# A delta-rule attention kernel with two feed-forward layers: the prologue of its first group on seven PSUM banks, x of the second layer in a buffer of its own, and group 1's key products kept in one piece

## What is computed

```python
def _attn_ref(q, k, v, beta):            # 4 x 8 heads, 768 steps, head size 48
    k_n = k / (np.linalg.norm(k, axis=-1, keepdims=True) + 1e-06)
    state = np.zeros((B, H, D, D))
    for t in range(S):
        kt, vt, bt = (k_n[:, :, t], v[:, :, t], beta[:, :, t, None])
        y[:, :, t] = np.einsum('bhd,bhde->bhe', q[:, :, t], state)
        v_old = np.einsum('bhde,bhd->bhe', state, kt)
        state = state + bt[:, :, :, None] * np.einsum('bhd,bhe->bhde', kt, vt - v_old)
    return y

x = heads side by side                   # 3072 tokens x 384
h = np.maximum(x @ w_in, 0.0)            # 384 -> 2048
x = h * h @ w_out                        # 2048 -> 384
gate = 1.0 / (1.0 + np.exp(-(x @ w_gate)))   # 384 -> 1536
y = gate * (x @ w_val) @ w_out2          # 1536 -> 384
```

## Time and profile before

| | us |
|---|---|
| median of 3 runs | 1003.74 |
| the runs | 1003.34 to 1004.78 |
| profiled execution, device time | 1005.03 |
| its span (first to last instruction) | 1003.3 |
| PE busy | 951.6 |
| DVE busy | 657.3 |
| ACT busy | 513.2 |

### The profile page before, as it was taken

How to read it: one execution, slowest core, us unless ns; L and a number is a source line. 1 busy time by engine, 2 the same in 40 slices (tenths; PEclk the granted TensorE clock), 3 DMA queues, 4 the chain that set the end, 5 groups by cost and what they waited for, 6 DMA issues and landing times.

```text
span 1003.3 us, 24593 instructions
## 1 busy us (share of the span) xinstructions
PE 951.6 (95%) x10354; PEld 523.5 (52%) x10354; DVE 657.3 (66%) x1261; ACT 513.2 (51%) x898; POOL 13.2 (1%) x27
## 2 busy tenths in 40 slices
PE   2876999999999999999999989999999999999998
PEld 1464465465456556546544435555555555555554
DVE  6978957957875794795334674575666665756745
ACT  4874666666476575646649943323233333232332
POOL 0000000000000000000000000000000000000000
PEclk7867999999999999999999999999999999999999
DMA  9516015115104201400215010010010010010000
GB/s 311 123 35 127 2 34 111 49 31 123 42 3 97 64 34 35 95 33 3 96 36 211 7 63 1 2 63 0 0 63 0 0 63 0 22 41 0 32 1 32
DMA packets 21001, 52.23 MB, mean 52 GB/s; under 512 B 2672, under 2 KB 12912, under 8 KB 20528
## 3 DMA queue, kind: packets, MB, share of 16 engines
q1 hardware_dynamic: 20320, 50.60, 18.1%
q10 hardware_dynamic: 592, 0.33, 0.2%
HBM read 41.48 MB, written 9.44 MB: 51 GB/s over the span
## 4 chain that ended last, share of the span: by engine, by line
PE 87%; DVE 6%; issue 3%; ACT 2%; DMA 1%; SPq 0%; POOL 0%; DVEq 0%; POOLq 0%
PE psum L673 74%; PE psum L587 3%; PE psum L518 1%; PE psum L544 1%; DMA raw_a<-in_w_in 1%; PE psum L531 1%; PE psum L574 1%; PE psum L602 1%; PE psum L556 1%; ACT w L900 1%; PE psum L616 1%; DVE attn L1192 1%; PE psum L483 1%; ACT w L806 1%; DVE work L1234 1%
## 5 line engine op out<-in xcount | busy, mean ns | idle before, releaser
L673 PE MATMUL psum<-work,w 128*128 128x512 f16 x1728 | 389.3, 382 | 12.2 <-issue 6.2
L673 PE MATMUL psum<-work,attn 128*128 128x512 f16 (+1 forms) x1836 | 367.6, 360 | 0.0
L673 PEld LDWEIGHTS psum<-work,attn 128*128 128x128 f16 x1836 | 179.5, 98 | 182.6 <-DVE work L1234 1.3
L673 PEld LDWEIGHTS psum<-work,w 128*128 128x128 f16 x1728 | 164.9, 98 | 209.3 <-issue 13.6
L806 ACT ACTIVATE work<-work 128x512 f16<-128x512 f32 (+1 forms) x264 | 155.7, 624 | 154.5 <-DVE work L1402 151.5
L1402 DVE SCALAR_TENSOR_TENSOR work<-psum,work 128x512 f32<-128x512 f32 x72 | 49.7, 691 | 134.5 <-PE psum L673 120.3
L1214 DVE SCALAR_TENSOR_TENSOR work<-work 128x512 f16<-128x512 f16 x96 | 66.2, 690 | 61.3 <-ACT work L806 59.6
L806 ACT ACTIVATE work<-psum,scal 128x512 f32<-128x512 f32 x90 | 60.1, 682 | 81.7 <-PE psum L673 81.6
L806 ACT ACTIVATE attn<-psum 64x384 f32<-64x384 f32 (+5 forms) x160 | 65.9, 441 | 66.3 <-PE psum L544 34.9
L806 ACT ACTIVATE work<-psum 128x512 f32<-128x512 f32 x96 | 57.1, 595 | 64.6 <-PE psum L673 63.3
L806 ACT ACTIVATE w<-w 128x1024 f16<-128x1024 f32 x36 | 38.0, 1057 | 72.6 <-DVE w L1418 72.6
(11 more groups left out here) (112 smaller groups left out, 713.7 us busy)
## 6 DMA issues: line engine op xcount, KB each, us to landing
attn<-in_kt SPq DMA_DIRECT2D x24, 192.0 KB, 4.4
attn<-in_v SPq DMA_DIRECT2D x24, 192.0 KB, 4.7
attn<-in_kn SPq DMA_DIRECT2D x24, 192.0 KB, 3.9
x_spill<-work SPq DMA_DIRECT2D x6, 768.0 KB, 3.4
xt<-x_spill SPq DMA_DIRECT2D x6, 768.0 KB, 5.0
attn<-in_qt SPq DMA_DIRECT2D x20, 192.0 KB, 4.3
y_out<-work SPq DMA_DIRECT2D x5, 768.0 KB, 3.6
work<-in_w_out SPq DMA_DIRECT2D x1, 3072.0 KB, 24.2
```

Of the source, the lines that this page charges most:

```text
L673: m = mm(dst, x, z, start=first and i == 0, stop=last and i == len(a) - 1)
```

## The change

- **Banks.** In stage 0 all fills but group 1's kk choose among seven banks (5, 6, 7, 2, 3, 4, 1), always the one that was filled longest ago; later stages and group 1's kk keep three. Banks 1 to 4 also serve the pieces of w_in's low part, so the first attention fill in each shared bank waits until all 12 pieces are copied out (`PIECE_SHARED`).
- **Group 1's key products.** Chunk by chunk, one product of 64 rows per pair instead of two of 32 (`HALVED` is empty). They stand between the pieces: 8 pieces, chunk 0, 2 pieces, chunk 1, 2 pieces. Read out in one piece each before (128x512), they now take four instructions per bank, as group 0's do.
- **Order of stage 0.** qk of chunk 0 ahead of mid; mid, off and `place_e` chunk by chunk; qk of chunk 1 is filled at step 9 and read at step 11. `cut_out`, `cut_small` and `first_weights_out` move. Twenty-five fillers stand behind five named fills instead of eight single ones ahead of fills.
- **x of group 0.** Its maximum is taken per chunk. ACT writes the three high parts, DVE only the low ones.
- **Loads.** SP issues group 1's keys ahead of v, q and k of group 0.
- **Stages 1 to 5.** Places move by a few steps, and so do the elimination columns.
- **Stage 6.** The second layer's weights are prepared in blocks 0 to 13 instead of 0 to 15, and its first x is split at block 12 into a buffer of its own (`x2_hi`, `x2_lo`, in the attention's memory), without the wait for the last `hidden`. The second layer reads x from there throughout.

```diff
+NB_FIRST = 7
-PLACE = dict(rows=6, scale_v=8, mid=(8, 11), off=(10, 14), qk=(-4, 10), ks=(8, 15), dr=(11, 16), grow=(13, 20), xt=(18, 21), xmax=23, xscale=27, xsplit=31, kk=(3, 5), lanes=14, norm=15, start=15)
+PLACE = dict(rows=7, scale_v=7, mid=(8, 11), off=(10, 15), qk=(-3, 10), ks=(7, 15), dr=(11, 17), grow=(13, 23), xt=(19, 25), xmax=26, xscale=27, xsplit=31, kk=(4, 5), lanes=7, norm=13, start=13)
+    _n = NB_FIRST if _s == 0 and (_kind, _g) != ("kk", 1) else NB
+    _b = min(range(_n), key=lambda b: _last[b])
...
-HALVED = (1,)
+HALVED = ()
-REST_FIRST = 12
+REST_AT = {OPEN: (0, 1, 2, 3, 4, 5, 6, 7), 0: (8, 9), 1: (10, 11)}
-WARM_AHEAD = ("mid", "off", "qk", "ks", "dr")
+WARM_BEHIND = {("mid", 0, 0): 4, ("mid", 1, 1): 1, ("dr", 1, 1): 4, ("su", 1, 1): 2, ("xt", 1, 1): 14}
...
-        a_bank = [psum[:, b, :] for b in (5, 6, 7)]
+        a_bank = [psum[:, b, :] for b in (5, 6, 7, 2, 3, 4, 1)]
...
+        x2_hi, x2_lo = (xs2[:, i * KC * TOK:(i + 1) * KC * TOK].rearrange("p (k t) -> p k t", k=KC) for i in (0, 1))
...
             def open_fill(*f):
+                if f in PIECE_SHARED:
+                    pe.wait_ge(w_lo_done, REST_PIECES)
...
+            def first_high_parts():
+                act.wait_ge(x_scaled, 5)
+                act.wait_ge(w_small_done, 1)
+                act.wait_ge(w_out_done, 1)
+                for kc in range(KC):
+                    run(x_hi[:, kc], xt32[:, TOK * kc:TOK * (kc + 1)], scale=cell(X + 2)).then_inc(x_cut, 1)
...
             def second_weights(k):
-                if k == 14:
+                if k == 10:
                     scale_x2(0)
...
+                if k == 12:
+                    split_x(x2_split, GROUPS, x2_hi, x2_lo)
...
-                    if s == GROUPS and step == place(s, "xsplit") + 1:
-                        dve.wait_ge(h_full, N1 * GROUPS)
-                        split_x(x2_split, GROUPS)
```

More of the change, by code:

```diff
@@ L137, in column_steps @@
     start, end = place(g - 1, "start") + 1, place(g, "rows")
-    steps = [(g - 1, step) for step in range(start, STEPS)]
+    steps = [(g - 1, step) for step in range(start, STEPS if g > 1 else place(0, "xsplit"))]
     steps += [(g, step) for step in range(0, end)]
@@ L654, in attention @@
                         turn(g, c, x)
+                    if s == 0:
+                        keep_clock(WARM_BEHIND.get((kind, c if kind not in ("mid", "off") else x, x), 0) if g == 0 else 0)
             def rest_of_first(n):
@@ L710, in stage @@
                     attention(s, step)
-                    if s == 0 and step == OPEN:
-                        for n in range(REST_FIRST):
-                            rest_of_first(n)
-                    for n in range(REST_FIRST, REST_PIECES):
-                        if s == 0 and step == place(0, "rest")[n - REST_FIRST]:
+                    if s == 0:
+                        for n in REST_AT.get(step, ()):
                             rest_of_first(n)
@@ L990, in stage @@
                         weight_root(1, WO)
-                        for n in range(REST_FIRST):
-                            cut_rest_first(n)
-                    if s == 0 and step == 0:
-                        place_e(0)
-                    for n in range(REST_FIRST, REST_PIECES):
-                        if s == 0 and step == place(0, "rest")[n - REST_FIRST]:
+                    if s == 0:
+                        for n in REST_AT.get(step, ()):
                             cut_rest_first(n)
@@ L1002, in stage @@
                             cut_small(n)
-                    if s < GROUPS - 1 and step == place(s, "norm"):
+                    if s < GROUPS - 1 and step == place(s, "norm" if s else "root"):
                         root_k(s + 1)
@@ L1342, in stage @@
                         scale_v(s)
-                    for f in FILL_AT.get((s, step), []):
+                    for f in READ_AT.get((s, step), []):
                         evacuate(*f)
+                    if s == 0 and step == place(0, "first_max"):
+                        max_of_chunk(0)
                     if chain and step == place(s, "xmax"):
```

161 lines of the change are left out of this document (102 added, 59 removed).

## The result

The changed kernel takes **995.1 us** (median of 6 runs, 994.0 to 999.2); the kernel before, run beside it, took 1003.86 (6 runs, 1002.6 to 1004.8). The ratio is 0.9919, with an interval of 0.9907 to 0.9932: 7 to 9 us faster. The profiled execution took 994.02, with a span of 992.2 instead of 1003.3. It was the fastest of its kernel, and that of before (1005.03) was slower than all six runs of its own, so the 11.1 us between the two traces are about 2.3 more than the medians show.

The account below looks back on a forecast made before the run. PE was taken to bound the kernel from the first `hidden` on, so the end moves with that start and seam losses: -4.6 - 0.4 + 0.3 + 0.2 = -4.5, from 1003.74 to 999.2; range 993.0 to 1003.3.

Parts of the forecast that it names:

- First qk at 49.2: Prologue: qk waits for all 12 pieces paced by ACT, starting 4.5 earlier; longer key read-out costs 2.8 on the path.
- qk to su of chunk 0: Prologue: PE's clock decides; 21.9 to 71.1 at the lower level, 13.6 with pauses to 62.8 at the upper.
- From su to the first `hidden`: Prologue: 7.0 to 7.7 to dr of chunk 1, 7.4 to 8.1 to the last xt, then 6.0.
- The clock: Prologue: PE near clock 0.5 for 13 to 17 us from 49 or 53 on.
- 90.0 for the first `hidden`: End of the prologue: taken between 88.6 and 92.0 for low spells of 13 and 17 us; 4.6 earlier.
- Rival 1: The clock holds through the prologue: first `hidden` at 85.1, -10.2 in all, 993.5; chance 0.15.
- Rival 2: Slower: the low spell lasts to the first `hidden`, at 97.9, later by 3.3; 1007.5; chance 0.08.
- Start of stage 1: First five blocks' worth: 12.7 becomes 11.5 if the clock holds, otherwise unchanged; -0.4, ends -1.2 and 0.
- Stages 1 to 5: More columns and later rows on DVE in stage 1 add waits, some go at the next seam; +0.3.
- Stage 6: The 3.38 wait goes, new idle times of 0.6, 1.9 and 3.1 come; +0.2; the 2.0 may lower the clock, +1.5.
- rival 3: No difference: low spell of 17 us or again in chunk 1, and stage 6's idle times lower the clock; 1004.4; chance 0.20.

Follow-up runs that it names:

- halved_keys: The changed kernel with group 1's key products in halves of 32 rows again, read out in one instruction per bank; ratio 0.9911 to the kernel before.
- spread_late_split: The changed kernel with stage 6's weights spread evenly, x's maximum at block 13 and its split behind the last hidden; ratio 0.9861 to the kernel before.
- s6_spread: The changed kernel with the second layer's weights spread evenly over stage 6, x's maximum at block 9, split at 10; ratio 0.9861 to the kernel before.
- more_fillers: The changed kernel with 27 instead of 14 fillers behind the last transposes and 8 behind chunk 0's; ratio 0.9904 to the kernel before, one run left out.
- old_places: The changed kernel with the kernel before's table of steps for stages 1 to 5; ratio 0.9939 to the kernel before.
- before_fillers: The kernel before with three fillers instead of one at eight places in stage 0 and 23 more behind the last transposes; ratio 1.0001 to the kernel before.
- s6_old: The changed kernel with stage 6 scheduled as in the kernel before, but x in its own buffer; ratio 0.9919 to the kernel before.

## Why the prediction was right, and where it was short

The forecast was 999.2, faster by 4.5; measured were 995.1, faster by 8.8. The sign, the range and the places held, the size was half.

1. **First qk at 49.2.** It came at 48.79, behind the last piece's copy, with 1.65 of idle time, and in all kernels with this order and wait between 48.6 and 50.4. The sum over ACT held. What it called a price, 2.8 us of longer read-out on the path, is answered by PE's shorter products, as halved_keys shows: no net loss.
2. **qk to su of chunk 0: the step that failed.** I gave 62.8 without and 71.1 with the low spell. Three traces with the same prologue have, before su is done, no low spell (spread_late_split), one of 6.8 us (the changed kernel) and one of 17.1 us (s6_spread): the next product starts at 63.2, 65.0 and 67.8. The upper end was right to 0.4, the lower too high by 3.3. I had put all 22 us of the stretch at the lower level and called it a spell of 17 us, with su at 1.7 where the clock was back for its second half and it took 1.1. And PE's pauses, which I had added at the upper level only, are what the lower level hides:

```profile
50.30:67.40 17.10, 13.88 (x605) 12.30 (x601) 16.12 (x30) 15.40 (x26) 0.00 (x0) 1.00 0.19 44
```

```profile
50.30:67.40 17.10, 17.10 (x451) 14.79 (x450) 12.85 (x19) 12.43 (x23) 0.00 (x0) 0.50 0.02 4
```

   These are the same stretch of spread_late_split and of s6_spread (columns as in the earlier trace rows): at full clock PE was idle for 3.2 of it, at half clock for none. Half the clock over 17 us cost 4.6 us (0.3 of them from the later start of qk), not 8.3.

   Two of the three pauses that I took from the earlier trace rows I had also read wrongly, as time in which PE waits for nothing. The profile says "issue" there, but both end 0.10 behind an end on ACT: 53.74 behind the read-out of mid (53.64), and 65.22 behind ACT's second copy out of dr (65.12), which stood behind the two pieces of w_out of the earlier trace rows:

```profile
64.14 1.49 ACT L806 ACTIVATE attn<-psum 64x384 f32<-64x384 f32 x3
```

   ACT doesn't slow with PE's clock: these copies take 1.49 here, at the lower level, and 1.49 at 73.40 in the changed kernel, at the upper one. That is why the lower level hides such pauses, and why fillers can't shorten a chain that runs through ACT.
3. **From su to the first `hidden`.** Forecast 22.3 or 20.9, by the clock; measured 21.2 in the changed kernel and in s6_spread alike.
4. **The clock.** I took a spell of 13 to 17 us; it was 6.8 in the profiled execution, 17.1 in another with the same prologue. The forecast's 90.0 for the first `hidden` is above that of all four traces with this prologue (85.5 to 89.0), so even with the spell that I assumed the prologue gained 5.6, and with the shorter one 8.4. Rival 1, in which the clock holds, gave 85.1 and 993.5, and came nearest, which is luck: the clock did not hold. The spell at 57.9 in the changed kernel began 0.2 behind the end of a pause of 0.92, but the same code ran without a fall there in spread_late_split, behind pauses of 0.65, 0.98 and 1.04. By the Trainium skill (TensorE: Matmul & The Clock Gate, "HAM oscillation — how this bites in real kernels") bursts that are broken by waits start cold; these traces agree only at times. Rival 2, a low spell that lasts to the first `hidden`, is not seen in any trace of this order.
5. **Start of stage 1.** Forecast -0.4, measured -0.3. The clock fell at 85.2 in the changed kernel; where it held (more_fillers), the wait of 1.31 appeared in place of the forecast 1.4.
6. **Stages 1 to 5: the other step that failed.** +0.3 was forecast, -1.9 measured in stages 2 and 5, of which old_places gives 1.4 to the places; 0.5 is a difference between two executions. I had worked out new waits at the seam of stage 1 (one came, 0.62 at 174.56, where 0.9 was forecast) and left alone what the new places do to the columns ahead of a rest. The waits of 0.47 and 0.62 at 192.87 and 445.44 had been in the trace of before; I filed them as short, and asked of none of them whether its cause stays. old_places, where both are back, shows that they were the places'.
7. **Stage 6.** Forecast idle times 0.6, 1.9, 0.6, 2.0 and 0.5, sum +0.2; measured 0.55, 1.68, 0.51, 1.83 and 0.21, sum 0.0. The step held, and so did its warning: the wait of 1.8 did not pull the clock down in any of the seven traces that have it.
8. **No difference, by rival 3**, needed the clock to fall again in chunk 1 and in stage 6. Neither happened.

Of the 8.4 us ahead of the first `hidden` the traces give 4 to 7 to the order. It is 7.0 from before_fillers to the changed kernel, both with 6.8 us of low clock in the stretch. It is 5.6 from before to s6_spread, both with 17.1, but before has a second spell at 83.4: from the second half of yy of chunk 1 to the first `hidden` it took 11.3 where before_fillers took 9.8, so that some 4.1 are left, an estimate. The rest is the clock of the profiled executions. The ratios, which don't rest on single traces, split the gain in the same way: with the old places the kernel still gains 6.1 us (0.9939), and as stage 6 gained nothing (s6_old), these lie in the prologue and the start of stage 1; three banks alone take 5.8 of the whole away again.

## What to carry to other kernels

When a preparation competes with a steady loop, divide the slack of each engine per step and spread the pieces by it. The 5 us that s6_spread found were visible in the trace of before as one wait of 3.38 and the 1.5 of low clock behind it, and the change moved them to four places because it pressed the same pieces into fewer blocks.

A low clock in a stretch of short products with pauses isn't worth its ratio: lay the stretch out twice, and let the slower products swallow the pauses. Where the profile names no releaser, look for an end on another engine just ahead before calling it a pause. And take every wait of the trace, however short, and ask whether the change moves what stands ahead of its releaser.
